# Four tiles declared after another one: the SBUF addresses of `act_t`, `hid_t`, `hi`, `lo` and `xT` in a fused convolution and two-layer gated MLP

## The reference

```
w   = softmax(weight)                          # 8 heads x 7 taps, causal convolution, 24 channels a head
a   = sum_k w[h, k] * x_padded[s + k]          # per sequence, 6 zeros ahead of it
b   = (sigmoid(a @ w_gate) * (a @ w_val)) @ w_out1      # 192 -> 1536 -> 192
out = relu(b @ w_in2) ** 2 @ w_out2                     # 192 -> 2048 -> 192
```

## Time and profile before

| What | Value |
|---|---|
| Median of 3 runs | 2385.3 us (2383.76 to 2386.93) |
| The profiled execution | 2385.3 us |
| Its span, first to last instruction | 2383.1 us |
| TensorE (PE) busy | 2351.4 us, 99% |
| TensorE weight loads (PEld) busy | 2119.0 us, 89% |
| VectorE (DVE) busy | 1824.3 us, 77% |
| ScalarE (ACT) busy | 1162.3 us, 49% |
| GpSimd (POOL) busy | 181.9 us, 8% |
| DMA queue of the data | 16.9% of 16 engines |

### The profile page before, as it was taken

The page is one execution under the profiler, slowest core; times in us unless marked ns, Lnnn a source line. Parts: engine busy times, 40 slices in busy tenths (PEclk is TensorE's granted clock), DMA queues, the critical chain, the costliest instruction groups (busy, mean ns, idle before and its releaser), DMA issues.

```text
span 2383.1 us, 54234 instructions
## 1 busy us (share of the span) xinstructions
PE 2351.4 (99%) x20880; PEld 2119.0 (89%) x20880; DVE 1824.3 (77%) x3468; ACT 1162.3 (49%) x2208; POOL 181.9 (8%) x164
## 2 busy tenths in 40 slices
PE   6999999999999999999999999999999999999998
PEld 5898998889899989998998888899989888998987
DVE  6777787777787877877777878778777787787755
ACT  3545454454544454544455444455445454454544
POOL 3300000000010000000000000001000000000110
PEclk9999999999999999999999999999999999999999
DMA  5211111111111111111111111111111111111110
GB/s 133 61 48 29 40 48 31 46 29 42 46 38 39 43 28 46 48 31 46 29 42 46 31 46 32 38 46 48 31 46 29 40 48 31 46 29 42 41 39 19
DMA packets 99901, 99.39 MB, mean 42 GB/s; under 512 B 8736, under 2 KB 86048, under 8 KB 99872
## 3 DMA queue, kind: packets, MB, share of 16 engines
q1 hardware_dynamic: 99856, 98.99, 16.9%
q10 hardware_dynamic: 16, 0.00, 0.0%
HBM read 19.27 MB, written 12.58 MB: 13 GB/s over the span
## 4 chain that ended last, share of the span: by engine, by line
PE 98%; DVE 1%; ACT 0%; issue 0%; DMA 0%; POOL 0%; SPq 0%; ACTq 0%; DVEq 0%
PE hp L400 36%; PE hp L401 18%; PE acc L466 17%; PE acc L471 11%; PE acc L467 9%; PE acc L472 6%; DVE y L815 1%; DMA stage<-in_moe_w_val_dram 0%; PE hp L506 0%; PE hp L507 0%; PE hp L515 0%; DVE hid_t L767 0%; POOL wo L358 0%; DMA moved<-z_parts 0%; SPq L263 0%
## 5 line engine op out<-in xcount | busy, mean ns | idle before, releaser
L400 PE MATMUL hp<-xs,w 64*128 64x512 f32 x5760 | 1407.1, 388 | 13.3 <-DVE hid_t L767 5.5
L401 PE MATMUL hp<-xs,w 64*128 64x512 f32 x5760 | 1406.9, 388 | 0.0
L400 PEld LDWEIGHTS hp<-xs,w 64*128 64x128 f32 x5760 | 1060.0, 185 | 121.5 <-DVE hid_t L767 7.4
L401 PEld LDWEIGHTS hp<-xs,w 64*128 64x128 f32 x5760 | 1060.0, 185 | 23.6
L781 DVE TENSOR_TENSOR lo<-hid_t,hi 128x512 fp32r<-128x512 f32 x896 | 617.1, 689 | 7.8
L625 ACT ACTIVATE act_t<-hp 128x512 f32<-128x512 f32 x384 | 230.0, 599 | 674.0 <-PE hp L400 674.0
L771 DVE TENSOR_TENSOR hid_t<-act_t 128x512 f32<-128x512 f32 x512 | 381.6, 746 | 228.4 <-ACT act_t L628 228.1
L466 PE MATMUL acc<-hi,wo 64*128 64x512 f32 x1792 | 549.5, 386 | 0.0
L467 PE MATMUL acc<-hi,wo 64*128 64x512 f32 x1792 | 549.4, 386 | 0.0
L767 DVE TENSOR_TENSOR hid_t<-hp,act_t 128x512 f32<-128x512 f32 x384 | 265.1, 690 | 246.1 <-ACT act_t L625 237.8
L628 ACT ACTIVATE act_t<-hp 128x512 f32<-128x512 f32 x512 | 302.7, 598 | 297.4 <-PE hp L401 180.0
(11 more groups left out here) (69 smaller groups left out, 1897.8 us busy)
## 6 DMA issues: line engine op xcount, KB each, us to landing
xs<-xs SPq DMA_DIRECT2D x160, 256.0 KB, 3.8
xs<-y_rest SPq DMA_DIRECT2D x128, 128.0 KB, 3.1
out_dram<-stage SPq DMA_DIRECT2D x32, 384.0 KB, 2.6
xin<-in_x_dram SPq DMA_DIRECT2D x30, 384.0 KB, 4.2
moved<-y_parts SPq DMA_DIRECT2D x32, 128.0 KB, 2.2
moved<-z_parts SPq DMA_DIRECT2D x64, 64.0 KB, 2.0
stage<-in_moe_w_out_dram SPq DMA_DIRECT2D x7, 384.0 KB, 5.0
stage<-in_moe_w_in_dram SPq DMA_DIRECT2D x12, 128.0 KB, 3.0
```

The costliest lines, as they stand in the source:

```text
L400: low = pe.matmul(hp[:, 2 * pair, :], w[lower, wk, c], xs[lower, xk, :], start=s, stop=e)
L401: up = pe.matmul(hp[:, 2 * pair + 1, :], w[upper, wk, c], xs[upper, xk, :], start=s, stop=e)
```

## The change

One declaration is moved. `xT` was declared behind `lo`, and now it stands ahead of `act_t`:

```diff
--- before
+++ after
@@ -71,11 +71,11 @@
         acc_up = sb("acc_up", [P, 2, N])
         xin = sb("xin", [P, B, D])
 
+        xT = sb("xT", [P, G, HALO + P])
         act_t = sb("act_t", [P, 2, N])
         hid_t = sb("hid_t", [P, 4, N])
         hi = sb("hi", [P, RING, N], F32R)
         lo = sb("lo", [P, RING, N], F32R)
-        xT = sb("xT", [P, G, HALO + P])
         taps = sb("taps", [P, 2, K])
         soft_w = sb("soft_w", [H, K])
         exp_w = sb("exp_w", [H, K])
```

## The result

The changed kernel takes 2421.53 us (median of 4 runs, 2420.87 to 2423.99), the kernel before 2384.53 us (median of 4, 2383.48 to 2386.93). The ratio is 1.0155, with a 95% interval of 1.0138 to 1.0173. The change costs 37 us. The forecast was no change, with a chance of 0.86. That was wrong: the forecast range ended at 2392 us. The time is the one that the first rival gave at its outer price, though its condition turned out to be another one, as the experiments show.

The account below looks back on a forecast made before the run. TensorE, full from 85 to 2374 us, was taken as the bound. Prices for TensorE's reads, VectorE's and ScalarE's work, `xT` and DMAs were all zero, so the sum of 0 us left 2385.3 us, range 2380 to 2392 us.

Parts of the forecast that it names:

- the first rival: L466 to L472: TensorE's stream pays for starts at 32 modulo 128; 2396 to 2421 us, nearly all of 0.08.
- What bounds the kernel: From 85 to 2374 us TensorE is busy for 2288.96 of 2289 us and waits for nobody to speak of.
- Each nanosecond of a pair is worth 4.5 us: 4480 pairs streaming `hi` and `lo`, about 1016 us, all on the path that sets the end.
- Step (a): TensorE reading `hi` and `lo` as moving operand, 4480 pairs: price taken as zero, outer end 36 us.
- The bound from VectorE's taps (8 ns): Taps 1 and 4 take 739 and 747 ns; the whole 8 ns on each `hi` or `lo` pair gives 36 us.
- The rule on 16-byte lines: SBUF is read in 16-byte lines, each cross costs; 3232 is 202 whole lines, so the move costs nothing.
- Step (b): VectorE's and ScalarE's work on the four moved tensors: price zero; without cover, 1% of VectorE would be 18 us.
- Step (c): `xT`'s move, only the first convolution (8 to 21 us) on the path: zero, plus or minus 1.4 us.
- Step (d): DMAs: none reads or writes one of the five moved tensors; price zero.
- the 1.07 ns: Price per pair of L466 to L472 from which the slower rival decides: 4.8 us over 4480 pairs.
- The second rival: `hi` or `lo` and `wo` weights sharing a remainder costs each pair; the change removes it: 2374 us, within 0.06.
- The third: VectorE slows by the new places until TensorE waits in the middle; about 2390 us if 5 us, chance 0.01.

Follow-up runs that it names:

- g3: Kernel before with a 32-byte tensor ahead of `act_t`, so `act_t`, `hid_t`, `hi`, `lo` and `xT` start at 32 modulo 128: 2431.19 us.
- g4: Kernel before with `soft_w` (32 bytes) between `hid_t` and `hi`, so only `hi`, `lo` and `xT` start at 32 modulo 128: 2432.31 us.
- g1: Changed kernel plus 96 bytes of filling behind `xT`, so `act_t`, `hid_t`, `hi` and `lo` start at 0 modulo 128 again: 2385.63 us.
- e5_all_at_32: Kernel before with `soft_w` (32 bytes) ahead of `w1`, so weights, `xs`, `hi`, `lo` and `xT` move together, keeping their distances: 2385.43 us.
- h1: Kernel before with filling ahead of `hi`, so `hi` and `lo` start 128 bytes higher; `act_t`, `hid_t`, `xs` and weights stay: 2424.87 us.
- e8_lo_at_32: Kernel before with `soft_w` between `hi` and `lo`, so only `lo` and `xT` behind it start at 32 modulo 128: 2403.39 us.

## Why the prediction was wrong

**What bounds the kernel** was right, and it is why a change that moves no instruction could cost 37 us: TensorE is full from 85 us on, so each nanosecond of a pair is on the path. "Each nanosecond of a pair is worth 4.5 us" held for the pairs of `hi` and `lo`.

**Step (a) failed.** It took zero "because the rows of TensorE itself are nearer than those of another engine". Those rows couldn't tell. They range over many regions and slots, but all weights, `xs`, `hi` and `lo` have the same remainder modulo 256, and every slice and slot keeps it. The quantity that matters had one single value in the whole trace. I took the spread over places that were alike for a test of places in general. Measured in its place: 6.8 ns a pair, with 1.3 ns more on the `xs` pairs by carry-over, which the step didn't have.

The bound from VectorE's taps (8 ns) gave an outer end of 36 us, which hits the measured 37. That is luck. The taps' 739 and 747 ns come from another engine, and the chip's loss depends on the distance to the weights, which the taps don't have. In the changed kernel VectorE's work keeps its durations (682 against 683 ns for L781), so that mechanism isn't the same.

**The rule on 16-byte lines** was weighed in the same step: "SBUF — State Buffer" in the Trainium skill, section Specifications. Its answer, zero for a move by whole lines, is not what was measured. Moves by 16, 32, 64 and 128 bytes are whole lines and cost 31 to 47 us, and a start inside a line (4 bytes, 56.5 us) cost no more than 96 bytes (57.4 us).

**Step (b)** was right. L781 has its old median, VectorE 1824.4 us for 1824.3, and g3 and g4, with and without `act_t` and `hid_t` moved, lose 45.9 and 47.0 us. **Step (c)** was right: the first 40 us are the same, and g1 with `xT` in its new place loses nothing. **Step (d)** was right.

**The rivals.** The first named the right place (L466 to L472, 4480 pairs) and had the time 2421 us at its outer price, but the wrong variable: a start at 32 modulo 128. `e5_all_at_32` has just that for all operands and is as fast as before. Its sign, that the pairs of L400 keep their pace, came out only in part: 228.1 ns for 226.8. And the 1.07 ns that it called a single extra line or beat is the time of 2.4 columns, at the measured 226.7 ns for 512. The second rival had the right variable, the relation between `hi` or `lo` and the weights, and the wrong sign: it took the common remainder for a cost, and it is what makes pairs fast. The third didn't happen.

**The numbers.** A chance of 0.86 for no change was too sure. The trace held no row for the new state, and for an engine that is full for 2289 of 2385 us (96%) both bounds of an unknown cost should have stayed in the range. The range cut them off at 1.5 ns a pair.

**What remains open.** The experiments show which distances are slow, not what inside the chip does it. Not settled are why 64 bytes costs less than 32 or 96, how much of it comes from a pair's own weights and how much from those loaded beside it, whether streams of neighbours disturb each other without the weights, and why the disturbance lasts for so long (with 128, in h1, the first ten `xs` pairs behind a border took 227.7 to 233.1 ns but for one). A distance of 256 modulo 512 was fast once (g1). Other multiples were not tried apart.

## What to carry to other kernels

When a trace shows a cost to be the same everywhere, ask first which values of the unknown it has seen. Here thousands of matmuls over 200 KB had one remainder modulo 256. In a kernel that TensorE fills with pairs like these, keep the start of each moving operand and of all weights at one remainder modulo 256 bytes, and round up behind a tensor of odd size (`xT` with 3216 bytes): 96 bytes of filling were worth 1.5%. A declaration moved, added or resized ahead of such tensors changed the time here by 0.8 to 2.8% with no instruction changed. Only this kernel's shapes and types were run (pairs of 64 rows, 512 columns, fp32r), so for others the advice is something to try and not shown.

## What the runs showed of the hardware

- With a 64-row pair of 512 columns in fp32r and its next weights being loaded, pairs follow at 226.7 ns when the moving operand and the weights have the same start modulo 256 bytes. When these differ, the pairs concerned follow at 231 to 236 ns on the mean of a kernel, by the distance. A difference of 4 bytes is enough (236.2 ns).
- The operands' common remainder doesn't matter: 128 and 160 modulo 256 both gave 2385 us.
- The same remainder of the difference gives the same time: 2421.5 and 2421.0 us for 160, and 2431.2 and 2431.0 us for 32.
- Slow pairs hand the disturbance on to aligned ones behind them, for three pairs in the changed kernel and for eight in `g4_hi_lo_at_32`, and it then dies out. It isn't always so: in `e8_lo_at_32` the `xs` pairs behind took 225.8 to 227.1 ns.
- VectorE and ScalarE, which read and write the same tensors, showed no change: 682 for 683 ns at the median of L781.
